# Attention and a gated MLP on one core: the product of the probabilities with V in full fp32, in two 64-column halves of TensorE's array, instead of split fp32r products

## The chip, the cores and the metric

The kernel runs on one core of one Trainium2 chip (trn2). The metric is device time in microseconds (us). TensorE (PE in the profile) multiplies, ScalarE (ACT), VectorE (DVE) and GpSimd (POOL) work on tiles, and SyncE (SP) only issues DMAs.

## What is computed

```python
# q, k, v: [4, 8, 576, 64]; w_in: [512, 2048]; w_out: [2048, 512]
q_rot, k_rot = rotate(q), rotate(k)                 # rotary embedding
scores = q_rot @ k_rot.T / sqrt(64)                 # per head, 576 x 576
attn = exp(scores - rowmax); attn = attn / (rowsum + 1e-9)
x = (attn @ v), heads side by side                  # [2304 tokens, 512]
h = x @ w_in
out = (h * tanh(softplus(h))) @ w_out               # [2304, 512]
```

## The kernel before, in words

**Attention.** The 32 heads go through a software pipeline, one head per step. Each engine works through a list written out by hand (`PE_STEP`, `ACT_STEP`, `DVE_STEP`, `POOL_STEP`). A piece such as `V0-3` is a kind, a number and a shift: in step n it handles head n-3. Each engine takes its pieces strictly in this order, so a piece that waits on a semaphore holds back all that stand behind it.

- On TensorE, K0 to K3 transpose q and k (L566, into `ps_t`). S0 to S4 are the scores of one tile of 128 queries against all keys (L580, four fp32r matmuls of 288 columns, into `ps_s`). T0 to T7 transpose the probabilities (L598, fp32, into one of the three banks of `ps_t`), and V0 to V7 are the product with V (L617, into `ps_pv`).
- On ScalarE, K copies q and k out of `ps_t` (L742), E is the exponential with row sums (L752), and H rounds a transposed group of P to fp32r, `ph` (L764).
- On VectorE, M is the row maximum (L897), L is the remainder `pl` = P - `ph` (L908, and L905 for the last, half-filled key tile), and K copies a part of q and k (L892).
- X copies the product with V from `ps_pv` to `xt`: 256 columns on VectorE (L918), 320 on ScalarE (L774).
- On GpSimd, R is the rotary embedding (L439 to L446), Q splits q and k into two fp32r parts (L452 to L457), C splits V (L466, L468), and B keeps the row sums (L474).

**The product with V.** P and V are each split into two fp32r parts. The two parts of V stand side by side as 128 stationary columns, so one matmul gives the product with both; 18 matmuls (nine of 256 queries, nine of 320) make a head. The part with V's remainder comes out on partitions 64 to 127, both halves go to DRAM, and the MLP adds them up (`sum_x`, L501).

**Banks.** A group T needs a bank of `ps_t` that the third piece before it (of K or T) has been copied out of: `wait_bank`.

**MLP.** Nine blocks of 256 tokens. `load_x` and `load_r` fetch x and the reciprocals of the row sums; GpSimd adds the two halves (L501), scales (L506) and splits (L511, L513); `hidden` is the first product (L681 to L683), `project` the second (L701 to L703). GpSimd's first block comes right behind its last pieces of attention and eight splits of `w_in` (L518, L520).

Of the kernel before, what the change touches and what calls it, by code (L numbers as in the profile page):

```python
# [32 lines left out]
P = 128  # L33
# [5 lines left out]
D = 64  # L39
# [10 lines left out]
LAST_GROUP = (2, 7)  # L50
WIDTH = tuple(len(tiles) * CHUNKS[chunk][1] for chunk, tiles in GROUPS)
GROUP_COL = tuple(sum(WIDTH[:g]) for g in range(NG))
# [4 lines left out]
def order(text):  # L57
# [66 lines left out]
def attention_mlp(nc, q, k, v, w_in, w_out, rope_cos, rope_sin, ident, out):  # L124
# [4 lines left out]
    xt_d = nc.dram_tensor("x_transposed", [2, KC, P, TOKENS], F32).ap()  # L129
# [3 lines left out]
    with ExitStack() as top:  # L133
# [19 lines left out]
        v_hi = sem("v_hi")  # L153
        v_split = sem("v_split")
# [31 lines left out]
        x_summed = sem("x_summed")  # L186
# [46 lines left out]
        v_raw = sb1("v_raw", [P, NT, D])  # L233
        v_st = sb1("v_st", [P, 2, NT, 2, D], F32R)
# [52 lines left out]
        def _(sp):  # L287
# [13 lines left out]
            def load_v(h):  # L301

                if due(h):
                    sp.wait_ge(v_split, h)
                head = v_d[bass.ds(h, 1), :, :]
                sp.dma_start(v_raw[:, 0:4, :],
                             head[:, 0:FULL, :].rearrange("a (t p) d -> p (a t) d", p=P)).then_inc(v_loaded, 16)

                for half in range(2):
                    sp.dma_start(v_raw[half * TAIL:half * TAIL + TAIL, 4, :],  # L310
                                 head[:, FULL:S, :].rearrange("a p d -> p (a d)")).then_inc(v_loaded, 16)

            def store_x(i, e):

                sp.wait_ge(x_taken_v, 2 * i + e + 1)
                sp.wait_ge(x_taken_a, 2 * i + e + 1)
                for a in range(2):
                    dst = xt_d[a, bass.ds(i % 4, 1), e * D:e * D + D, bass.ds((i // 4) * S, S)]
                    sp.dma_start(dst.rearrange("c p s -> (c p) s"), xt[a * D:a * D + D, e, :]
                                 ).then_inc(x_stored[e], 16)  # L320
# [33 lines left out]
            def load_x(b):  # L354

                if due(b):
                    sp.wait_ge(xb_split, b)
                for a, dst in enumerate((x_raw, x_more)):
                    sp.dma_start(dst[:], xt_d[a, :, :, bass.ds(b * TB, TB)].rearrange("c p t -> p c t")
                                 ).then_inc(x_loaded, 16)  # L360

            def load_r(b):

                sp.wait_ge(x_summed, b + 1)
# [37 lines left out]
            sp.wait_ge(pv_done, NG * HEADS)  # L402
# [22 lines left out]
        def _(pool):  # L425
            nc.gpsimd.memset(first[TAIL:P, 0, :, 4, :], 0.0)
            nc.gpsimd.memset(qk_raw[TAIL:P, :, 4, :], 0.0)
            nc.gpsimd.memset(prob[TAIL:P, 0, 4, :], 0.0)
            nc.gpsimd.memset(sums[TAIL:P, :, :], 1.0).then_inc(pads_cleared, 1)
# [30 lines left out]
            def split_v(h, e):  # L460
                pool.wait_ge(v_loaded, 48 * (h + 1))

                if due(NG * (h - 1)):
                    pool.wait_ge(pv_done, NG * (h - 1))
                pool.sem_inc(pool_through, 1)
                nc.gpsimd.tensor_scalar(v_st[:, e, :, 0, :], v_raw[:], 1.0, 1.0, ALU.mult, ALU.mult).then_inc(v_hi, 1)  # L466
                pool.wait_ge(v_hi, h + 1)
                nc.gpsimd.tensor_tensor(v_st[:, e, :, 1, :], v_raw[:], v_st[:, e, :, 0, :].bitcast(F32),  # L468
                                        ALU.subtract).then_inc(v_split, 1)

# [57 lines left out]
            sum_x(0)  # L528
# [3 lines left out]
            with pool.Fori(1, NB) as b:  # L532
                sum_x(b)
# [4 lines left out]
        def _(pe):  # L538
            def wait_bank(slot, n):
# [5 lines left out]
                if kind == "T":  # L545
                    pe.wait_ge(pt_split, NG * head + k + 1)
# [54 lines left out]
            def p_times_v(h, e, g):  # L601
                chunk, tiles = GROUPS[g]
                nq = CHUNKS[chunk][1]
                pe.wait_ge(pt_split, NG * h + g + 1)
                if g == 0:
                    pe.wait_ge(v_split, h + 1)

                if g == 0:
                    if due(h):
                        pe.wait_ge(x_taken_a, h)  # L610
                elif g == 3:
                    pe.wait_ge(x_taken_v, h + 1)
# [17 lines left out]
            def step(i, e):  # L630
                slot = 0
                for kind, k, shift in PE_STEP:
# [13 lines left out]
                    elif real(h):  # L646
                        if kind == "S":
                            scores(h, parity, k)
                        else:
                            p_times_v(h, parity, k)  # L650
# [14 lines left out]
            pe.wait_ge(pt_split, NG * HEADS)  # L665
# [63 lines left out]
        def _(act):  # L729
# [27 lines left out]
            def p_hi(h, g):  # L757
                w, col = WIDTH[g], GROUP_COL[g]
                act.wait_ge(pt_done, NG * h + g + 1)

                if due(h):
                    act.wait_ge(pv_done, NG * (h - 1) + g + 1)
                rows = slice(0, P) if GROUPS[g][1] != (4,) else slice(TAIL, P)
                nc.scalar.activation(ph[rows, col:col + w], ps_t[rows, SLOT_OF["T", g] % NTB, 0:w],  # L764
                                     ACT.Copy).then_inc(pt_hi, 1)

            def take_x(pair, h, e):

                first, nq = CHUNKS[1]
                act.wait_ge(pv_done, NG * h + LAST_GROUP[1] + 1)  # L770

                if due(pair):
                    act.wait_ge(x_stored[e], 32 * pair)
                nc.scalar.activation(xt[:, e, first:first + nq], ps_pv[:, 0:nq], ACT.Copy).then_inc(x_taken_a, 1)  # L774

            def step(i, e):
                for kind, k, shift in ACT_STEP:
                    h, parity = 2 * i + e + shift, (e + shift) % 2
                    if real(h):
# [4 lines left out]
                        elif kind == "H":  # L784
                            p_hi(h, k)
                        else:
                            take_x(i + (e + shift) // 2, h, parity)
# [48 lines left out]
            act.wait_ge(pv_done, NG * HEADS)  # L836
# [25 lines left out]
        def _(dve):  # L862
# [37 lines left out]
            def p_lo(h, g):  # L900
                w, col, bank = WIDTH[g], GROUP_COL[g], SLOT_OF["T", g] % NTB
                dve.wait_ge(pt_hi, NG * h + g + 1)
                if GROUPS[g][1] == (4,):

                    nc.vector.tensor_tensor(ph[0:TAIL, col:col + w], ps_t[TAIL:P, bank, 0:w],  # L905
                                            ph[TAIL:P, col:col + w].bitcast(F32), ALU.subtract).then_inc(pt_split, 1)
                else:
                    nc.vector.tensor_tensor(pl[:, col:col + w], ps_t[:, bank, 0:w],  # L908
                                            ph[:, col:col + w].bitcast(F32), ALU.subtract).then_inc(pt_split, 1)

            def take_x(pair, h, e):

                first, nq = CHUNKS[0]
                dve.wait_ge(pv_done, NG * h + LAST_GROUP[0] + 1)
# [3 lines left out]
                nc.vector.tensor_copy(xt[:, e, first:first + nq], ps_pv[:, 0:nq]).then_inc(x_taken_v, 1)  # L918
# [17 lines left out]
            def step(i, e):  # L936
                for kind, k, shift in DVE_STEP:
                    h, parity = 2 * i + e + shift, (e + shift) % 2
                    if real(h):
# [4 lines left out]
                        elif kind == "L":  # L944
                            p_lo(h, k)
# [3 lines left out]
                    if isinstance(h, int):  # L949
# [4 lines left out]
                        elif kind == "L" and k == 5 and h == HEADS - 1:  # L954
# [86 lines left out]
```

## Time and profile before

| | |
|---|---|
| median of 3 runs | 747.14 us (746.15 to 747.2) |
| the profiled execution | 747.9 us, span of the core 745.9 us |
| TensorE busy | 714.6 us, 96% |
| ScalarE / VectorE / GpSimd busy | 552.6 / 462.1 / 371.3 us |
| mean granted TensorE clock | 0.998 |
| attention | to about 333 us; from 100 to 290 us twenty steps of 9.5 us |
| MLP | from 336.2 us on |

TensorE's matmuls are pipelined, so an entry's duration is longer than the distance to the next one: what a matmul costs in a stream is the distance between starts. The chain of work gives such times directly: each of its pieces ends where the next begins.

### The profile page before, as it was taken

What the parts mean: (1) busy time and instruction counts of PE and PEld (TensorE: products, weight loads), DVE (VectorE), ACT (ScalarE), POOL (GpSimd) and SP (SyncE); (2) the same over time, 40 slices, a digit from 0 to 9 for tenths busy, and PEclk for the clock granted to TensorE, in tenths of its full rate; (3) what the DMA queues carried; (4) which work ended last, traced back from release to release, by engine and by line L of the source; (5) the groups of instructions that cost most, each with busy time, mean ns of one, the idle gap of its engine ahead of it and who ended that gap; (6) DMA issues with size and microseconds to landing.
All of it is one profiled execution on the core that took longest, in us unless ns stands there. A gap on an engine that the chain in (4) does not pass through costs nothing.

```text
span 745.9 us, 16092 instructions
## 1 busy us (share of the span) xinstructions
PE 714.6 (96%) x5098; PEld 666.3 (89%) x5098; DVE 462.1 (62%) x665; ACT 552.6 (74%) x999; POOL 371.3 (50%) x373
## 2 busy tenths in 40 slices
PE   1899999999999999979999999999999999999998
PEld 1799999999999999879899988999988999988996
DVE  4688888888888888975764533343453442533341
ACT  1799999999999999876777576656657557466653
POOL 4999999999999999971411303112030221301000
PEclk9999999999999999999999999999999999999999
DMA  4136633333333333256200201012020200200000
GB/s 86 41 70 194 193 80 78 77 80 79 76 80 81 81 81 81 81 167 222 84 29 29 85 29 58 28 47 66 28 84 0 84 28 28 84 28 0 0 28 28
DMA packets 89956, 52.30 MB, mean 70 GB/s; under 512 B 65456, under 2 KB 79408, under 8 KB 89936
## 3 DMA queue, kind: packets, MB, share of 16 engines
q1 hardware_dynamic: 89936, 52.03, 25.5%
q8 instruction: 12, 0.20, 0.1%
q14 instruction: 8, 0.07, 0.0%
HBM read 37.78 MB, written 14.23 MB: 70 GB/s over the span
## 4 chain that ended last, share of the span: by engine, by line
PE 85%; POOL 6%; issue 3%; DVE 3%; ACT 2%; DMA 1%; SPq 0%; POOLq 0%
PE ps_t L598 10%; PE ps_s L580 9%; PE ps_pv L617 9%; PE ps_h L681 9%; PE ps_y L701 9%; PE ps_h L683 9%; PE ps_h L682 9%; PE ps_y L702 9%; PE ps_y L703 9%; PE ps_t L566 5%; POOL qk_st L457 1%; POOL qk_st L455 1%; POOL win_lo L520 1%; DMA x_more<-reciprocals 1%; DMA sin_t<-rope_sin 0%
## 5 line engine op out<-in xcount | busy, mean ns | idle before, releaser
L989 DVE TENSOR_TENSOR h_sb<-h_sb,m_sb 128x1024 f32<-128x1024 f32 x36 | 57.0, 1583 | 198.5 <-ACT m_sb L823 198.5
L681 PE MATMUL ps_h<-xb_h,win_hi 128*128 128x256 f32 x576 | 163.7, 284 | 2.9 <-POOL xb_l L513 2.9
L682 PE MATMUL ps_h<-xb_l,win_hi 128*128 128x256 f32 x576 | 163.7, 284 | 0.0
L683 PE MATMUL ps_h<-xb_h,win_lo 128*128 128x256 f32 x576 | 163.7, 284 | 0.0
L752 ACT ACTIVATE prob<-ps_s,neg_max 128x576 f32<-128x576 f32 (+1 forms) x160 | 119.0, 743 | 12.9 <-POOL sum_all L474 8.9
L598 PE MATMUL ps_t<-id_f,prob 128*128 128x128 f32 x800 | 125.3, 275 | 0.7 <-DVE rt_early L934 0.3
L897 DVE TENSOR_REDUCE neg_max<-ps_s 128x1 f32<-128x576 f32 (+1 forms) x160 | 119.4, 746 | 5.7 <-PE ps_s L580 5.6
L580 PE MATMUL ps_s<-qkt 128*128 128x288 f32 x640 | 120.6, 311 | 1.9 <-ACT prob L752 1.3
L764 ACT ACTIVATE ph<-ps_t 128x320 fp32r<-128x320 f32 (+3 forms) x256 | 117.6, 473 | 4.8 <-PE ps_t L598 2.5
L681 PEld LDWEIGHTS ps_h<-xb_h,win_hi 128*128 128x128 f32 x576 | 111.2, 193 | 3.8 <-issue 3.2
L701 PE MATMUL ps_y<-wout_hi,gh 128*128 128x512 f32 x288 | 112.4, 390 | 1.0 <-DVE gl L999 1.0
L702 PE MATMUL ps_y<-wout_lo,gh 128*128 128x512 f32 x288 | 112.3, 390 | 0.0
L703 PE MATMUL ps_y<-wout_hi,gl 128*128 128x512 f32 x288 | 112.0, 389 | 0.0
L682 PEld LDWEIGHTS ps_h<-xb_l,win_hi 128*128 128x128 f32 x576 | 111.3, 193 | 0.6
L683 PEld LDWEIGHTS ps_h<-xb_h,win_lo 128*128 128x128 f32 x576 | 111.3, 193 | 0.0
L617 PE MATMUL ps_pv<-ph,v_st 128*128 128x256 f32 (+1 forms) x320 | 106.5, 344 | 2.7 <-DVE xt L918 2.5
L908 DVE TENSOR_TENSOR pl<-ps_t,ph 128x320 fp32r<-128x320 f32 (+1 forms) x192 | 102.9, 551 | 6.2 <-ACT ph L764 0.8
L819 ACT ACTIVATE m_sb<-m_sb 128x1024 f32<-128x1024 f32 x36 | 38.2, 1060 | 90.3 <-DVE m_sb L984 90.3
L511 POOL TENSOR_SCALAR xb_h<-x_raw 128x1024 fp32r<-128x1024 f32 x9 | 9.5, 1054 | 181.2 <-PE ps_h L683 181.0
L598 PEld LDWEIGHTS ps_t<-id_f,prob 128*128 128x128 f32 x800 | 93.7, 140 | 4.8 <-DVE pl L908 0.6
L580 PEld LDWEIGHTS ps_s<-qkt 128*128 128x128 f32 x640 | 92.2, 192 | 3.2 <-ACT prob L752 1.7
L566 PE MATMUL ps_t<-id_r,qk_st 128*128 128x128 f32 x480 | 61.6, 252 | 19.0 <-DVE id_r L884 15.0
(63 smaller groups left out, 1303.8 us busy)
## 6 DMA issues: line engine op xcount, KB each, us to landing
x_transposed<-xt SPq DMA_DIRECT2D x64, 144.0 KB, 2.4
x_raw<-x_transposed SPq DMA_DIRECT2D x9, 512.0 KB, 4.0
x_more<-x_transposed SPq DMA_DIRECT2D x9, 512.0 KB, 4.9
x_more<-reciprocals SPq DMA_DIRECT2D x18, 256.0 KB, 3.8
v_raw<-v_in SPq DMA_DIRECT2D x32, 128.0 KB, 2.2
win_raw<-w_in SPq DMA_DIRECT2D x4, 1024.0 KB, 5.6
wout_raw<-w_out SPq DMA_DIRECT2D x4, 1024.0 KB, 9.4
y_out<-y_sb SPq DMA_DIRECT2D x8, 512.0 KB, 2.8
```

The lines of the kernel that those rows point to most:

```text
L580: mm = nc.tensor.matmul(ps_s[:, buf, part, 0:S // 2], qkt[:, e, stack, t * P:t * P + P], qkt[:, e, 2, part * (S // 2):(part + 1) * (S // 2 ...
L598: mm = nc.tensor.transpose(bank[:, col:col + P], src, id_f[:])
L617: mm = nc.tensor.matmul(ps_pv[:, 0:nq], vT, part[:, col:col + nq], start=(kt == 0 and lo == 0), stop=(kt == 4))
L681: nc.tensor.matmul(o, wh, xb_h[:, c, :], start=(c == 0), stop=False)
L682: nc.tensor.matmul(o, wh, xb_l[:, c, :], start=False, stop=False)
L683: mm = nc.tensor.matmul(o, wl, xb_h[:, c, :], start=False, stop=(c == KC - 1))
L701: nc.tensor.matmul(o, g_h, wout_hi[:, f, :], start=(f == 0), stop=False)
L702: nc.tensor.matmul(o, g_h, wout_lo[:, f, :], start=False, stop=False)
L703: mm = nc.tensor.matmul(o, g_l, wout_hi[:, f, :], start=False, stop=(f == FT - 1))
L752: nc.scalar.activation(prob[0:rows, e, t, :].rearrange("p (a k) -> p a k", a=2), ps_s[0:rows, (5 * e + t) % 2, :, 0:S // 2], ACT.Exp, bias ...
L764: nc.scalar.activation(ph[rows, col:col + w], ps_t[rows, SLOT_OF["T", g] % NTB, 0:w], ACT.Copy).then_inc(pt_hi, 1)
L897: nc.vector.tensor_reduce(neg_max[0:rows, e, t:t + 1], ps_s[0:rows, (5 * e + t) % 2, :, 0:S // 2], AX.XY, ALU.max, negate=True).then_inc(m ...
```

## The change

P stays one fp32 tensor `pt`, and V is loaded from DRAM straight into `v_st`. All V pieces of a head become one, `V0`: for each of five key tiles, two fp32 matmuls with 64 stationary columns, one for queries 0 to 287 (output partitions 0 to 63), one for queries 288 to 575 (partitions 64 to 127). `V0` waits until all eight groups T of its head are copied. Each group is copied once: groups 0 and 5 on ScalarE, the other six on VectorE (all H now). X is one copy of 288 columns on VectorE. C, the second store of x and `sum_x` are gone. The key tile of the last 64 keys has zeros on its first 64 rows of `v_st`.

```diff
-PE_STEP = order("V0-3 K0 V1-3 K1 S1-1 K2 T0-2 K3 V2-3 S2-1 T1-2 V3-3 V4-3 T2-2 S3-1 T3-2 V5-3 T4-2 "
-                "V6-3 S4-1 T5-2 V7-3 T6-2 T7-2 S0")
-ACT_STEP = order("E0 K2+1 H0-1 E1 H1-1 K3+1 H2-1 E2 H3-1 H4-1 E3 H5-1 X1-2 H6-1 E4 H7-1 K0+2")
-DVE_STEP = order("M4-1 L5-2 L6-2 M0 L7-2 K1+1 M1 X0-2 L0-1 M2 L1-1 M3 L2-1 L3-1 L4-1")
-POOL_STEP = order("Q0+3 C0+1 B0 R0+4")
+PE_STEP = order("K0 K1 V0-3 S1-1 K2 T0-2 K3 S2-1 T1-2 T2-2 S3-1 T3-2 T4-2 S4-1 T5-2 T6-2 T7-2 S0")
+ACT_STEP = order("E0 K2+1 H0-1 E1 K3+1 E2 E3 H5-1 E4 K0+2")
+DVE_STEP = order("M4-1 H6-2 M0 H7-2 K1+1 M1 X0-2 M2 H1-1 H2-1 M3 H3-1 H4-1")
+POOL_STEP = order("Q0+3 B0 R0+4")
...
             def step(i, e):
                 n = 2 * i + e
                 if real(n - 2):
                     store_x(i - 1, e)
-                if real(n + 1):
-                    load_v(n + 1)
+                if real(n - 1):
+                    load_v(n - 1, (e - 1) % 2)
...
-            def p_times_v(h, e, g):
...
-                for j, kt in enumerate(tiles):
-                    vT = v_st[:, e, kt, :, :].rearrange("p a d -> p (a d)")
-                    col = GROUP_COL[g] + j * nq
-                    for lo, part in enumerate((ph, pl) if kt < 4 else (ph,)):
-                        mm = nc.tensor.matmul(ps_pv[:, 0:nq], vT, part[:, col:col + nq],
-                                              start=(kt == 0 and lo == 0), stop=(kt == 4))
+            def p_times_v(h, e):
+                wait_taken(h, NG - 1)
+                wait_taken(h, ACT_GROUPS[-1])
+                pe.wait_ge(v_loaded, 32 * (h + 1))
+                if due(h):
+                    pe.wait_ge(x_taken, h)
+                for kt in range(NT):
+                    for side in range(2):
+                        mm = nc.tensor.matmul(ps_pv[side * D:side * D + D, 0:S // 2], v_st[:, e, kt, :],
+                                              pt[:, kt, side * (S // 2):(side + 1) * (S // 2)],
+                                              start=(kt == 0), stop=(kt == 4))
                 mm.then_inc(pv_done, 1)
...
+            def take_p(h, g):
+                chunk, tiles = GROUPS[g]
+                first, nq = CHUNKS[chunk]
+                dve.wait_ge(pt_done, NG * h + g + 1)
+
+                if due(h):
+                    dve.wait_ge(pv_done, h)
+                src = ps_t[:, SLOT_OF["T", g] % NTB, 0:WIDTH[g]].rearrange("p (j q) -> p j q", q=nq)
+                nc.vector.tensor_copy(pt[:, tiles[0]:tiles[-1] + 1, first:first + nq], src).then_inc(pt_taken_v, 1)
```

TensorE, from the end of one step of attention into the next, before (`ps_t<-id_f,prob` are transposes of P, `ps_t<-id_r,qk_st` those of q and k):

```order
L598 MATMUL ps_t<-id_f,prob 128x128 [waits pt_split]
L598 MATMUL ps_t<-id_f,prob 128x128 x2
L580 MATMUL ps_s<-qkt 128x288 [waits exp_done,kt_taken_v,kt_taken_a]
L580 MATMUL ps_s<-qkt 128x288 x3
L617 MATMUL ps_pv<-ph,v_st 128x256 [waits x_taken_a,v_split,pt_split]
L617 MATMUL ps_pv<-pl,v_st 128x256
L617 MATMUL ps_pv<-ph,v_st 128x256
L617 MATMUL ps_pv<-pl,v_st 128x256
L566 MATMUL ps_t<-id_r,qk_st 128x128 [waits qk_parts,pt_split]
L566 MATMUL ps_t<-id_r,qk_st 128x128 x3
```

The same place of the changed kernel:

```order
L574 MATMUL ps_t<-id_f,prob 128x128 [waits pt_taken_v]
L574 MATMUL ps_t<-id_f,prob 128x128 x2
L556 MATMUL ps_s<-qkt 128x288 [waits exp_done,kt_taken_v,kt_taken_a]
L556 MATMUL ps_s<-qkt 128x288 x3
L542 MATMUL ps_t<-id_r,qk_st 128x128 [waits qk_parts,pt_taken_a]
L542 MATMUL ps_t<-id_r,qk_st 128x128 x3
L542 MATMUL ps_t<-id_r,qk_st 128x128 [waits pt_taken_v]
L542 MATMUL ps_t<-id_r,qk_st 128x128 x3
L585 MATMUL ps_pv<-pt,v_st 64x288 [waits v_loaded,x_taken,pt_taken_a,pt_taken_v]
L585 MATMUL ps_pv<-pt,v_st 64x288 x9
L556 MATMUL ps_s<-qkt 128x288 [waits exp_done]
L556 MATMUL ps_s<-qkt 128x288 x3
```

The product with V stood in eight places of the step, each waiting for one group of P; now it stands in one, behind K1, and waits for the last group.

VectorE around the same point, before (the 64-row maximum is M4, the one behind it M0; L905 is the remainder of group 7):

```order
L897 TENSOR_REDUCE neg_max<-ps_s 64x1 [waits s_done]
L908 TENSOR_TENSOR pl<-ps_t,ph 128x320 [waits pt_hi] x2
L897 TENSOR_REDUCE neg_max<-ps_s 128x1 [waits s_done]
L905 TENSOR_TENSOR ph<-ps_t,ph 64x320 [waits pt_hi]
L892 CAST qkt<-ps_t 128x512 [waits s_done,kt_done]
L897 TENSOR_REDUCE neg_max<-ps_s 128x1 [waits s_done]
L918 COPY xt<-ps_pv 128x256 [waits pv_done]
```

and now:

```order
L857 TENSOR_REDUCE neg_max<-ps_s 64x1 [waits s_done]
L868 COPY pt<-ps_t 128x320 [waits pv_done,pt_done]
L857 TENSOR_REDUCE neg_max<-ps_s 128x1 [waits s_done]
L868 COPY pt<-ps_t 128x320 [waits pv_done,pt_done]
L852 CAST qkt<-ps_t 128x512 [waits s_done,kt_done]
L857 TENSOR_REDUCE neg_max<-ps_s 128x1 [waits s_done]
L876 COPY xt<-ps_pv 128x288 [waits pv_done]
```

The last group's piece kept its place behind M0; what waits for it on TensorE has moved.

## Rows read from the trace of the kernel before

**Rows 1.** Busy time of each engine in twenty steps (stretches; columns as headed).

```profile
core 0: us, PE busy (x) PEld busy (x) DVE busy (x) ACT busy (x) POOL busy (x), PEclk, DMA share, GB/s
100.00:290.00 190.00, 188.53 (x1560) 182.05 (x1559) 168.10 (x301) 177.41 (x441) 178.05 (x201) 1.00 0.35 79
```

**Rows 2.** Chain of work: shares of the span, then shares of 100 to 290 us.

```profile
PE 85%; POOL 6%; issue 3%; DVE 3%; ACT 2%; DMA 1%; SPq 0%; POOLq 0%
...
by line: PE ps_t L598 26.3%; PE ps_s L580 25.7%; PE ps_pv L617 24.6%; PE ps_t L566 14.0%; issue 6.9%; POOL qk_st L457 2.5%; POOLq L465 0.1%
```

**Rows 3.** Chain of work in one step: start us, us, what.

```profile
199.64 0.55 PE ps_pv L617 x4
200.19 0.29 PE ps_t L566 x4
...
203.19 0.58 PE ps_pv L617 x4
...
208.10 0.48 POOL qk_st L457
```

**Rows 4.** TensorE in order of time: start us, us, line, what, [idle before, releaser].

```profile
206.63 0.82 PE L598 MATMUL ps_t<-id_f,prob 128*128 128x128 f32 x6
207.21 0.77 PE L580 MATMUL ps_s<-qkt 128*128 128x288 f32 x4
207.82 0.28 PE L617 MATMUL ps_pv<-ph,v_st 128*128 128x256 f32 x1
...
208.17 0.28 PE L617 MATMUL ps_pv<-pl,v_st 128*128 128x256 f32 x1
208.62 0.54 PE L566 MATMUL ps_t<-id_r,qk_st 128*128 128x128 f32 x4 [0.17 <-POOL qk_st L457]
```

**Rows 5.** Groups by shape: count, busy us, mean ns, idle before.

```profile
L617 PEld LDWEIGHTS ps_pv<-ph,v_st 128*128 128x128 f32 x320 | 60.3, 188 | 4.0 <-issue 2.2 <-DVE ph L905 1.3
L908 DVE TENSOR_TENSOR pl<-ps_t,ph 128x320 fp32r<-128x320 f32 x128 | 59.1, 483 | 4.3
L897 DVE TENSOR_REDUCE neg_max<-ps_s 128x1 f32<-128x576 f32 x128 | 95.7, 747 | 4.9 <-PE ps_s L580 4.9
L752 ACT ACTIVATE prob<-ps_s,neg_max 128x576 f32<-128x576 f32 x128 | 95.3, 745 | 12.3 <-POOL sum_all L474 8.9 <-DVE neg_max L897 2.5
L764 ACT ACTIVATE ph<-ps_t 128x512 fp32r<-128x512 f32 x64 | 38.2, 597 | 2.4 <-PE ps_t L598 1.8
```

**Rows 6.** The page's group of all roundings of P on ScalarE.

```profile
L764 ACT ACTIVATE ph<-ps_t 128x320 fp32r<-128x320 f32 (+3 forms) x256 | 117.6, 473 | 4.8 <-PE ps_t L598 2.5
```

**Rows 7.** GpSimd's split of V in order of time.

```profile
208.52 0.47 POOL L466 TENSOR_SCALAR v_st<-v_raw 128x320 fp32r<-128x320 f32 x1
209.07 0.88 POOL L468 TENSOR_TENSOR v_st<-v_raw,v_st 128x320 fp32r<-128x320 f32 x1
```

**Rows 8.** Chain of work from attention into the MLP.

```profile
322.65 2.35 POOL x_raw L501
...
325.76 4.11 DMA x_more<-reciprocals
330.00 2.38 POOL x_raw L506
...
333.69 2.37 POOL xb_l L513
...
337.26 0.21 PE ps_h L682
...
341.05 0.12 PE ps_h L683
```

**Rows 9.** TensorE's first matmul of the MLP in order of time.

```profile
336.20 0.42 PE L681 MATMUL ps_h<-xb_h,win_hi 128*128 128x256 f32 x1 [2.89 <-POOL xb_l L513]
```

**Rows 10.** SyncE's DMA issues in order of time.

```profile
207.72 1.25 SPq L319 DMA_DIRECT2D x_transposed<-xt  x2
210.11 0.40 SPq L306 DMA_DIRECT2D v_raw<-v_in  x1
```

**Rows 11.** DMA issues of 100 to 290 us: count, KB each, median us from issue to landing.

```profile
v_raw<-v_in SPq DMA_DIRECT2D x20, 128.0 KB, 2.2
```

More of the change, by code:

```diff
@@ L49 @@
 NG = len(GROUPS)
-LAST_GROUP = (2, 7)
 WIDTH = tuple(len(tiles) * CHUNKS[chunk][1] for chunk, tiles in GROUPS)
-GROUP_COL = tuple(sum(WIDTH[:g]) for g in range(NG))
+ACT_GROUPS = (0, 5)
 NK = 4
@@ L299, in load_qk, with load_v @@
                                  head[:, FULL:S, :].rearrange("a p d -> p (a d)")).then_inc(loaded, 16)
-            def load_v(h):
-                if due(h):
-                    sp.wait_ge(v_split, h)
+            def load_v(h, e):
+                if due(h - 1):
+                    sp.wait_ge(pv_done, h - 1)
                 head = v_d[bass.ds(h, 1), :, :]
-                sp.dma_start(v_raw[:, 0:4, :],
+                sp.dma_start(v_st[:, e, 0:4, :],
                              head[:, 0:FULL, :].rearrange("a (t p) d -> p (a t) d", p=P)).then_inc(v_loaded, 16)
-                for half in range(2):
-                    sp.dma_start(v_raw[half * TAIL:half * TAIL + TAIL, 4, :],
-                                 head[:, FULL:S, :].rearrange("a p d -> p (a d)")).then_inc(v_loaded, 16)
+                sp.dma_start(v_st[TAIL:P, e, 4, :],
+                             head[:, FULL:S, :].rearrange("a p d -> p (a d)")).then_inc(v_loaded, 16)
             def store_x(i, e):
[L315 to L319, printed above, removed]
+                sp.wait_ge(x_taken, 2 * i + e + 1)
+                for side in range(2):
+                    dst = xt_d[bass.ds(i % 4, 1), e * D:e * D + D, bass.ds((i // 4) * S + side * (S // 2), S // 2)]
+                    sp.dma_start(dst.rearrange("c p s -> (c p) s"), xt[side * D:side * D + D, e, :]
                                  ).then_inc(x_stored[e], 16)
@@ L357, in load_x @@
                     sp.wait_ge(xb_split, b)
-                for a, dst in enumerate((x_raw, x_more)):
-                    sp.dma_start(dst[:], xt_d[a, :, :, bass.ds(b * TB, TB)].rearrange("c p t -> p c t")
-                                 ).then_inc(x_loaded, 16)
+                sp.dma_start(x_raw[:], xt_d[:, :, bass.ds(b * TB, TB)].rearrange("c p t -> p c t")
+                             ).then_inc(x_loaded, 16)
             def load_r(b):
-                sp.wait_ge(x_summed, b + 1)
+                if due(b):
+                    sp.wait_ge(xb_split, b)
                 for e in range(2):
@@ L538, in _, with wait_taken @@
         def _(pe):
+            def wait_taken(head, g):
+                mine = [x for x in range(NG) if (x in ACT_GROUPS) == (g in ACT_GROUPS)]
+                pe.wait_ge(pt_taken_a if g in ACT_GROUPS else pt_taken_v, len(mine) * head + mine.index(g) + 1)
             def wait_bank(slot, n):
@@ L545, in wait_bank @@
                 if kind == "T":
-                    pe.wait_ge(pt_split, NG * head + k + 1)
+                    wait_taken(head, k)
                 elif not real(head):
@@ L599, in p_turn @@
                 mm.then_inc(pt_done, 1)
-            def p_times_v(h, e, g):
[L602 to L612, printed above, removed]
-                for j, kt in enumerate(tiles):
-                    vT = v_st[:, e, kt, :, :].rearrange("p a d -> p (a d)")
-                    col = GROUP_COL[g] + j * nq
-                    for lo, part in enumerate((ph, pl) if kt < 4 else (ph,)):
-                        mm = nc.tensor.matmul(ps_pv[:, 0:nq], vT, part[:, col:col + nq],
-                                              start=(kt == 0 and lo == 0), stop=(kt == 4))
+            def p_times_v(h, e):
[5 more added lines that the diff above has]
+                for kt in range(NT):
+                    for side in range(2):
+                        mm = nc.tensor.matmul(ps_pv[side * D:side * D + D, 0:S // 2], v_st[:, e, kt, :],
+                                              pt[:, kt, side * (S // 2):(side + 1) * (S // 2)],
+                                              start=(kt == 0), stop=(kt == 4))
                 mm.then_inc(pv_done, 1)
@@ L663, in _ @@
                 step(n // 2, n % 2)
-            pe.wait_ge(pt_split, NG * HEADS)
+            wait_taken(HEADS - 1, NG - 1)
+            wait_taken(HEADS - 1, ACT_GROUPS[-1])
             turn_reciprocals(1, range(4), 0)
@@ L755, in exps @@
                                      accum_out=sums[0:rows, e, t:t + 1]).then_inc(exp_done, 1)
-            def p_hi(h, g):
-                w, col = WIDTH[g], GROUP_COL[g]
+            def take_p(h, g):
+                chunk, tiles = GROUPS[g]
+                first, nq = CHUNKS[chunk]
                 act.wait_ge(pt_done, NG * h + g + 1)
                 if due(h):
[L762 to L774, printed above, removed]
+                    act.wait_ge(pv_done, h)
+                src = ps_t[:, SLOT_OF["T", g] % NTB, 0:WIDTH[g]].rearrange("p (j q) -> p j q", q=nq)
+                nc.scalar.activation(pt[:, tiles[0]:tiles[-1] + 1, first:first + nq], src,
+                                     ACT.Copy).then_inc(pt_taken_a, 1)
             def step(i, e):
@@ L898, in row_max, with take_p @@
                                         ALU.max, negate=True).then_inc(max_done, 1)
[L900 to L909, printed above, removed]
+            def take_p(h, g):
+                chunk, tiles = GROUPS[g]
+                first, nq = CHUNKS[chunk]
+                dve.wait_ge(pt_done, NG * h + g + 1)
+                if due(h):
+                    dve.wait_ge(pv_done, h)
+                src = ps_t[:, SLOT_OF["T", g] % NTB, 0:WIDTH[g]].rearrange("p (j q) -> p j q", q=nq)
+                nc.vector.tensor_copy(pt[:, tiles[0]:tiles[-1] + 1, first:first + nq], src).then_inc(pt_taken_v, 1)
             def take_x(pair, h, e):
-                first, nq = CHUNKS[0]
-                dve.wait_ge(pv_done, NG * h + LAST_GROUP[0] + 1)
+                dve.wait_ge(pv_done, h + 1)
                 if due(pair):
                     dve.wait_ge(x_stored[e], 32 * pair)
-                nc.vector.tensor_copy(xt[:, e, first:first + nq], ps_pv[:, 0:nq]).then_inc(x_taken_v, 1)
+                nc.vector.tensor_copy(xt[:, e, :], ps_pv[:, 0:S // 2]).then_inc(x_taken, 1)
             def reciprocals(late):
@@ L953, in step @@
                             take_reciprocals(0)
-                        elif kind == "L" and k == 5 and h == HEADS - 1:
+                        elif kind == "H" and k == 6 and h == HEADS - 1:
                             reciprocals(1)
```

53 lines of the change are left out of this document (15 added, 38 removed).

## The prediction

> **What bounds the kernel now.** I read the busy times of a stretch in the middle of attention first. In twenty steps, 190 us, TensorE is busy for 188.5 us, GpSimd for 178.1, ScalarE for 177.4 and VectorE for 168.1 [rows 1]: four engines within a tenth of each other, with TensorE in front. The chain of work says which of them sets the end. Over the whole span it runs through TensorE for 85% and GpSimd for 6%; in the twenty steps 90.6% of it lies on TensorE and 9.5% on GpSimd's split of q and k and the issue time around it [rows 2]. The order of time shows why: after V's four matmuls TensorE stands still until GpSimd has finished L457, which ends at 208.58, and starts K0 at 208.62 [rows 3, 4]. The last V matmul began at 208.17 and the next instruction could have followed 0.12 us later, so about 0.3 us of a step of 9.5 us is a wait for GpSimd, and the rest is TensorE's own work. The MLP is TensorE's too, and the change leaves its matmuls alone.
>
> So the question is what TensorE's step costs afterwards: its own work, plus waits that stand in its queue.
>
> **TensorE's work.** Of the part of the chain that is on TensorE, the product with V has 24.6 of 90.6 [rows 2]: 0.27 of 9.5 us, or 2.6 us a step. That agrees with pieces of 0.55 and 0.58 us for four matmuls [rows 3]. The other pieces take 9.5 - 2.6 - 0.3 = 6.6 us, and none of them changes.
>
> The trace has no full fp32 product, so the ten new matmuls of 288 columns must be bounded. Four fp32r matmuls of 288 columns, S, take 0.61 us to the next start [rows 4], some 0.13 to 0.15 us each. If a full fp32 matmul cost no more, ten would take 1.3 to 1.5 us. Precision costs passes, though: fp32 transposes of P take 0.58 us for six, 0.097 us each [rows 4], where the fp32r ones of q and k take 0.29 us for four, 0.073 us each [rows 3]. Scaled from 128 to 288 columns, the fp32 price is 0.22 us, and ten make 2.2 us. The upper end is the kernel's own recipe: it gets fp32 from two parts of P times two parts of V, four partial products. Four fp32r products of 0.13 us are 0.53 us for each matmul, ten are 5.3 us; if the two halves run side by side in the array, 2.65 us. Two routes (one after another at the transposes' price, side by side at four products) give 2.2 and 2.65. I take 2.6 us, since the kernel's own way to fp32 needs all four products. The ends are 1.3 and 5.3.
>
> Changing between 128 and 64 columns may empty the array twice a step. A matmul of 0.28 us whose successor starts 0.12 us later [rows 4] overlaps 0.16 us, so this costs at most 0.3 us a step; it goes into the range.
>
> The Trainium skill, "FP8 and Floating Point Precision", TensorE Precision Notes, puts true fp32 at four passes through the array, high and low part of each operand. At 2.4 GHz that would be 4 x 288 columns, 0.48 us; "TensorEngine Tiling (Array Packing)", Theoretical Speedup, gives up to twofold for operands of at most 64 columns, so 2.4 us a head by both rules and 4.8 by the first alone. No row here shows either rule at work on a product.
>
> **What goes away elsewhere.** ScalarE's roundings of P are 117.6 us for 256 [rows 6], of which two of eight groups stay; it also loses X. GpSimd loses 0.47 + 0.88 us a step [rows 7], so it is done with q and k early, and TensorE's 0.3 us wait before K0 goes. All the rest of this relief lies beside TensorE's work and is worth nothing by itself: with ScalarE below 6.5 us and GpSimd near 8 us, TensorE is alone in front.
>
> **The wait that comes in.** V0 waits for H7, the copy of the last group of P, and H7 stands behind M0 on VectorE; M0 needs S0, which TensorE runs after T7. Count from S0's start. S0 takes 0.61 us to issue and ends at 0.77 [rows 4]. M0 takes 0.75, a copy of 320 columns about 0.48 (the nearest row is L908) [rows 5]: H7 is done at 2.0 us. TensorE has S0, K0 and K1 to do, 0.61 + 0.29 + 0.29 = 1.2 us, and stands still for 0.8 us. Before, V7 stood late in the next step and its group had several us. Behind the waiting V0 is everything: S1, and with it M1, E1 and the whole next round, so nothing takes the 0.8 us back.
>
> A smaller one stands before S3, which needs E1. On ScalarE, E1 is behind H0, and H0 needs T0. From S1's start: S1 0.6, K2 0.3, T0 0.4, its end 0.2, H0 0.6 and E1 0.75 [rows 5] are 2.85 us; TensorE has S1, K2, T0, K3, S2, T1 and T2, some 2.6 us. V2, V3 and V4 used to stand between these and cover it; now 0.2 to 0.4 us shows. I take 0.3.
>
> **V's load.** V is now fetched two steps later: on SyncE's queue it stands behind the store of the previous head's x, which needs X, which stands behind M1. From V0's end: S1, M1 and X, 0.77 + 0.75 + 0.48 = 2.0 us; two stores 1.25, two issues of V some 0.4 each [rows 10], gaps together perhaps 0.4; landing 2.2 [rows 11]; about 6.7 us. The next V0 starts 10.3 - 2.6 = 7.7 us after this one's end, so it is hidden, with 1 us to spare. In the last, short steps (head 31) 1 to 2 us of it can show.
>
> **Sum for a step.** 6.6 + 2.6 + 0.8 + 0.3 = 10.3 us against 9.5: +0.8 to 0.9. Steps 3 to 31 have both K and V; the first of them are still filling before and after, so I count 28: +24 us.
>
> **Into the MLP.** Before, GpSimd adds the halves of x (2.35 us), only then are the reciprocals asked for (4.1 us to land), and scaling and splitting run from 330.0 to 336.1 [rows 8]. Without the addition the reciprocals are there early, and the 6 us of splitting can start with the last exponential, which T3 to T7 and V0 of head 31 still follow. TensorE then goes on at once after its last transposes, where it stood still for 2.9 us [rows 9] and then ran at half clock, 0.21 us a matmul instead of 0.12 [rows 8], for about 16 matmuls, 1.5 us. Against these 4.4 us stands head 31's late V. I take -3 us.
>
> Total: 745.9 + 24 - 3 = 767 us of span. The profiled execution's time is 2.0 us above its span and 0.8 above the median, so 768 us for the median. A measurement of this kernel tells 0.2%, 1.5 us, from no change.
>
> **Rivals.**
>
> *The halves run one after another* at four products each: V takes 4.8 to 5.3 us, the step 12.5 to 13.0, +3.0 to +3.5 us for 28 steps, less 3: 828 to 842 us. For it: nothing in the trace shows two matmuls in the array at once, and a weight load of 0.19 us stands before each matmul [rows 5]; if ten of these are not hidden, that alone is 1.9 us. Against it: the two halves share no columns of the array and no partitions of the result, and the trace shows each matmul overlapping its neighbour by more than half of its duration (0.28 us long, 0.12 us apart [rows 4]), so entries behind one another do flow together. The Trainium skill, "TensorE: Matmul & The Clock Gate", The mechanism, says that a weight load overlaps matmuls in flight only where the row groups differ; here both halves use all rows, which speaks for this rival.
>
> *A full fp32 column is cheap* (faster than before): if ten matmuls take 1.3 us, the two waits of 1.1 us still stand, and the step is 6.6 + 1.3 + 1.1 = 9.0, -0.45 us for 28 steps and -3: 731 us. The point from which it decides: V below about 1.6 us a head. For it, the two prices of a transpose, 0.097 against 0.073, are not far apart; with the halves side by side that factor would give 1.1 to 1.3 us.
>
> *The waits are covered.* If VectorE or ScalarE's order lets the waits vanish, V at 2.6 us only replaces V at 2.6, the 0.3 us wait for GpSimd goes, and the time is 735 to 747 us. It needs H7 done within 1.2 us of S0's start, and M0 alone ends at 1.5.
>
> **Chances.** Forecast (V at 2.2 to 3.0 us with its waits) 0.60, giving 755 to 782. One after another 0.22. Cheap fp32 0.13. Waits covered 0.05, mostly faster. Slower 0.82, same 0.03, faster 0.15. The range leaves out the cheap case and reaches over the serial one: 745 to 855.
>
> **What the profile after would show.** TensorE's V matmuls 0.5 us apart in pairs with starts close together (or in a row, for the rival); idle time of about 0.8 us before V0 put down to VectorE's copy L868; GpSimd waiting over 2 us a step; steps of 10.3 us; the MLP beginning without a gap. The prediction is wrong if V's ten matmuls take under 1.6 us or over 3.5, or if V0 does not wait for L868.

## The result: slower by 5.5%, by the forecast mechanism, with almost twice the forecast size

| | before | changed |
|---|---|---|
| median | 747.13 us (746.15 to 747.2) | 787.6 us (786.75 to 788.66) |
| ratio | | 1.0546, 95% interval 1.0527 to 1.0564 |
| span of the profiled run | 745.9 us | 786.9 us |
| a step in the middle of attention | 9.52 us | 10.70 us |
| TensorE's first matmul of the MLP | 336.2 us | 378.3 us |

The forecast was 768 us, +21 us; the measurement is +40.5 us. All of it lies in attention: the MLP begins 42.1 us later and then takes 1 us less.

The busy times of the same stretch as [rows 1], 100 to 290 us of the changed kernel:

```profile
core 0: us, PE busy (x) PEld busy (x) DVE busy (x) ACT busy (x) POOL busy (x), PEclk, DMA share, GB/s
100.00:290.00 190.00, 176.24 (x1421) 147.89 (x1421) 124.76 (x230) 110.92 (x266) 133.21 (x142) 1.00 0.24 55
```

The three other engines lost 43 to 67 us of work in this stretch and are far from full. A part of that is only that fewer steps fit into it, 17.8 in place of 20; counted per step, ScalarE's work fell by 30% and VectorE's and GpSimd's by 16%. TensorE is not full either: 176 us of 190 where it had 188.5. An engine that was the bound now waits. What it waits for stands in the waits of this stretch (who, for whom, us in total, times, longest):

```profile
DVE neg_max L857 <- PE ps_s L556: 63.0, 36, 3.1
ACT qkt L712 <- PE ps_t L542: 60.1, 18, 3.4
POOL qk_st L442 <- PE ps_t L542: 52.4, 18, 3.0
...
PE ps_pv L585 <- DVE pt L868: 13.8, 18, 0.8
```

VectorE, ScalarE and GpSimd each wait some 3 us a step for TensorE, and TensorE waits 0.8 us a step for the copy of P, L868. In order of time, one V0 and what leads to it:

```profile
206.72 0.79 PE L556 MATMUL ps_s<-qkt 128*128 128x288 f32 x4
...
207.35 0.80 PE L542 MATMUL ps_t<-id_r,qk_st 128*128 128x128 f32 x8
207.55 0.76 DVE L857 TENSOR_REDUCE neg_max<-ps_s 128x1 f32<-128x576 f32 x1
...
208.23 0.48 DVE L868 COPY pt<-ps_t 128x320 f32<-128x320 f32 x1
...
208.95 2.65 PE L585 MATMUL ps_pv<-pt,v_st 128*64 128x288 f32 x20 [0.80 <-DVE pt L868]
...
211.53 0.80 PE L556 MATMUL ps_s<-qkt 128*128 128x288 f32 x4
```

S0 starts at 206.72, M0 at 207.55, H7 at 208.23 and ends at 208.71, V0 starts at 208.95. H7 is done 2.0 us after S0's start, as forecast; V0 follows 0.24 us later, which the forecast left out. V0 takes 2.65 us; the next S starts 2.58 us after it. The profile counts 20 entries for ten matmuls: a full fp32 matmul stands there as two instructions with a weight load each. The 20 weight loads of this V0 are busy for 1.61 us and lie inside its 2.65 us, so the rival's price for weight loads that are not hidden (1.9 us) does not show.

Then the end of attention. The last three V0 of the changed kernel, in order of time:

```profile
353.84 4.30 PE L585 MATMUL ps_pv<-pt,v_st 128*64 128x288 f32 x20 [6.69 <-DMA v_st<-v_in]
365.55 2.65 PE L585 MATMUL ps_pv<-pt,v_st 128*64 128x288 f32 x20 [1.86 <-DMA v_st<-v_in]
373.58 4.33 PE L585 MATMUL ps_pv<-pt,v_st 128*64 128x288 f32 x20 [1.80 <-DMA v_st<-v_in]
```

All three wait for V's load, the first for 6.7 us, and two of them take 4.3 us. The forecast had 1 to 2 us for the late load, at head 31 alone; the waits and the slow V0 come to far more. The stretches of the three V0 show why two are slow (the last number but two is the granted clock):

```profile
353.80:358.10 4.30, 4.26 (x21) 2.30 (x21) 0.00 (x0) 0.00 (x0) 0.00 (x0) 0.60 0.44 114
365.50:368.20 2.70, 2.65 (x21) 1.68 (x22) 0.00 (x0) 0.00 (x0) 2.50 (x2) 1.00 0.97 309
...
373.50:377.90 4.40, 4.32 (x21) 2.45 (x22) 0.00 (x0) 2.10 (x5) 0.00 (x0) 0.61 0.00 0
```

The clock granted to the first and the third is 0.60 and 0.61 on average, that is, for most of the stretch the lower level, 1.2 GHz, after waits of 6.7 and 1.8 us. The chain of work up to the first shows how the load came to be late:

```profile
347.31 0.48 DVE pt L868
347.80 0.79 DVE rt_early L892 x2
348.61 0.38 SPq L365
349.03 0.29 SPq L365
349.37 0.29 SPq L365
349.71 0.47 SPq L308
350.22 0.60 SPq L308
350.86 0.59 SPq L298
...
351.51 2.08 DMA v_st<-v_in
...
353.84 0.71 PE ps_pv L585
```

SyncE's program stores the reciprocals of the first 24 heads (L365) at this point, and these are transposed by TensorE just ahead of V0 of head 29. The load of V for that V0 (L298) stands behind the three stores and two stores of x (L308).

### The profile page after: what moved, and what is told of

Its sections match the earlier page's. It is cut to its first block, busy times and chain, and to the rows that moved or that the text cites. A ratio compares the mean times of both kernels' runs of the same rounds, so it can differ in the third digit from the quotient of the medians.

```text
span 786.9 us, 15331 instructions
## 1 busy us (share of the span) xinstructions
PE 731.0 (93%) x5162; PEld 641.2 (81%) x5162; DVE 404.6 (51%) x601; ACT 468.2 (59%) x775; POOL 304.9 (39%) x301
## 4 chain that ended last, share of the span: by engine, by line
PE 84%; DVE 4%; issue 3%; ACT 2%; DMA 2%; POOL 2%; SPq 1%; DVEq 0%; POOLq 0%
PE ps_s L556 12%; PE ps_pv L585 11%; PE ps_t L574 11%; PE ps_y L671 8%; PE ps_y L672 8%; PE ps_y L673 8%; PE ps_h L653 8%; PE ps_h L652 8%; PE ps_h L651 8%; PE ps_t L542 2%; DVE pt L868 2%; DMA v_st<-v_in 1%; DMA sin_t<-rope_sin 0%; DVE gh L955 0%; POOL part_s L431 0%
## 5 line engine op out<-in xcount | busy, mean ns | idle before, releaser
L722 ACT ACTIVATE prob<-ps_s,neg_max 128x576 f32<-128x576 f32 (+1 forms) x160 | 119.0, 744 | 34.1 <-DVE neg_max L857 34.0
L556 PE MATMUL ps_s<-qkt 128*128 128x288 f32 x640 | 126.7, 321 | 1.8 <-ACT prob L722 1.2
L712 ACT ACTIVATE qkt<-ps_t 128x512 fp32r<-128x512 f32 (+1 forms) x96 | 54.3, 566 | 117.9 <-PE ps_t L542 116.2
L585 PE MATMUL ps_pv<-pt,v_st 128*64 128x288 f32 x640 | 88.0, 422 | 32.0 <-DVE pt L868 21.1
L574 PE MATMUL ps_t<-id_f,prob 128*128 128x128 f32 x800 | 115.1, 278 | 0.3 <-ACT pt L735 0.3
L585 PEld LDWEIGHTS ps_pv<-pt,v_st 128*64 128x64 f32 x640 | 52.4, 141 | 55.9 <-issue 30.5
L574 PEld LDWEIGHTS ps_t<-id_f,prob 128*128 128x128 f32 x800 | 90.6, 141 | 8.3 <-DVE pt L868 2.0
L868 DVE COPY pt<-ps_t 128x320 f32<-128x320 f32 (+1 forms) x192 | 90.9, 501 | 0.8 <-PE ps_t L574 0.8
```

What stands on the lines that cost most here:

```text
L556: mm = nc.tensor.matmul(ps_s[:, buf, part, 0:S // 2], qkt[:, e, stack, t * P:t * P + P], qkt[:, e, 2, part * (S // 2):(part + 1) * (S // 2 ...
L574: mm = nc.tensor.transpose(bank[:, col:col + P], src, id_f[:])
L585: mm = nc.tensor.matmul(ps_pv[side * D:side * D + D, 0:S // 2], v_st[:, e, kt, :], pt[:, kt, side * (S // 2):(side + 1) * (S // 2)], start ...
L722: nc.scalar.activation(prob[0:rows, e, t, :].rearrange("p (a k) -> p a k", a=2), ps_s[0:rows, (5 * e + t) % 2, :, 0:S // 2], ACT.Exp, bias ...
L868: nc.vector.tensor_copy(pt[:, tiles[0]:tiles[-1] + 1, first:first + nq], src).then_inc(pt_taken_v, 1)
```

## The experiments

Each ran beside the kernel before; the ratios are to it. Its median was 747.22 us beside four of them (V loaded earlier, H7 first, the halves one after another, all orders changed) and 747.94 us beside the other four, so a difference between one of the first and one of the second four is good to about 1 us.

**V loaded one step earlier.** Head n's V is fetched in SyncE's step n, not n+1, and each of the two buffers has its own semaphore.

```diff
-                if real(n - 1):
-                    load_v(n - 1, (e - 1) % 2)
+                if real(n):
+                    load_v(n, e)
...
-                pe.wait_ge(v_loaded, 32 * (h + 1))
+                pe.wait_ge(v_loaded[e], 32 * (pair + 1))
```

> The changed kernel with each head's V loaded one step earlier on SyncE's queue, with a semaphore for each of the two buffers of V. Theory (the last three heads wait for V): V0 of heads 29, 30 and 31 no longer waits 6.7, 1.9 and 1.8 us for its load, and no V runs at half clock (4.3 us instead of 2.65, twice); about 10 to 12 us less than the changed kernel, 776 us; the steps in the middle stay at 10.7 us. Rival (the loads are late because the DMA queues are full, not because of their place in SyncE's order): under 3 us less.

Measured: 777.44 us (777.2 to 777.74), ratio 1.0403 (1.0386 to 1.042), 10.2 us below the changed kernel. The steps in the middle did not change. The last three V0:

```profile
347.18 2.65 PE L585 MATMUL ps_pv<-pt,v_st 128*64 128x288 f32 x20 [0.70 <-DVE pt L868]
356.29 2.65 PE L585 MATMUL ps_pv<-pt,v_st 128*64 128x288 f32 x20 [0.91 <-DVE pt L868]
364.17 2.65 PE L585 MATMUL ps_pv<-pt,v_st 128*64 128x288 f32 x20 [1.66 <-DVE pt L868]
```

None of them waits for a DMA, and none takes 4.3 us. The load was late by its place in SyncE's order, and the rival of full queues falls. Wait and duration together, head 29 gave back 7.6 us, head 30 1.0 us and head 31 1.8 us.

**H7 ahead of M0** on VectorE:

```diff
-DVE_STEP = order("M4-1 H6-2 M0 H7-2 K1+1 M1 X0-2 M2 H1-1 H2-1 M3 H3-1 H4-1")
+DVE_STEP = order("M4-1 H6-2 H7-2 M0 K1+1 M1 X0-2 M2 H1-1 H2-1 M3 H3-1 H4-1")
```

> The changed kernel with H7 ahead of M0 in VectorE's order, nothing else. Theory (V0 waits for the copy of the last group of P behind M0): the wait of 0.7 to 0.8 us before V0 goes, steps of 10.0 us instead of 10.7, 28 of them, 768 us. Rival (the wait moves: M0 comes 0.5 us later, and with it E0 and the rest of the round): steps stay above 10.4 us, 780 us or more.

Measured: 765.13 us (764.42 to 766.45), ratio 1.0241 (1.0224 to 1.0258), 22.5 us below the changed kernel. In the middle V0 no longer waits; the distance of two V0 is 217.27 - 207.42 = 9.85 us:

```profile
206.01 0.77 PE L556 MATMUL ps_s<-qkt 128*128 128x288 f32 x4
206.62 0.87 PE L542 MATMUL ps_t<-id_r,qk_st 128*128 128x128 f32 x8
207.42 2.65 PE L585 MATMUL ps_pv<-pt,v_st 128*64 128x288 f32 x20
...
217.27 0.95 PE L585 MATMUL ps_pv<-pt,v_st 128*64 128x288 f32 x6
```

One exchange of two pieces on an engine that is idle a third of the time took back more than half of the loss: 0.85 us a step. Two things of the load of V are mixed into the 22.5 us. V0 of head 31 runs at full clock here, 2.65 us in place of 4.33 (only head 29's is still slow, 4.38 us behind a wait of 6.46), and in the first 100 us three V0 now wait for their load, 1.8 us in all, which they do not in the next kernel, with V loaded earlier.

**Both together.**

> load_ahead and h7_first together. If both causes are separate, 777.4 - (787.6 - 765.1) = 755 us and steps of 9.85 us as in h7_first; if the waits of the last heads were partly the same time twice, 757 to 760 us. The distance to reordered (752.5 us) is then what the order on TensorE and ScalarE gives.

Measured: 754.25 us (753.81 to 756.66), ratio 1.0103 (1.0073 to 1.0133), steps of 9.84 us. The gains add up to within 1 us. In part that is chance: head 31's full clock (1.7 us) is gained by either edit alone and so only once by both, and the three early waits of the kernel with H7 first (1.8 us) go only with both.

**The halves one after another.** The loop over the halves outside, the one over key tiles inside; the same ten matmuls.

```diff
-                for kt in range(NT):
-                    for side in range(2):
+                for side in range(2):
+                    for kt in range(NT):
```

> The changed kernel with the two loops of V0 exchanged: five matmuls of the first half of the queries in the first 64 columns, then five of the second half in the others; the same ten matmuls. Theory (a full fp32 matmul of 288 columns takes 0.48 us, and 2.6 us for ten come from two halves side by side): V0 takes 5.0 us instead of 2.6, steps of 13.1 us, 32 times 2.4 us more, 864 us. Rival (nothing runs side by side, ten matmuls cost 0.26 us each one after another): no change, 787 us.

Measured: 834.05 us (833.61 to 835.66), ratio 1.1168 (1.1149 to 1.1187). V0 takes 4.12 us, clearly more than 2.65 and clearly less than the 5.0 of the theory. The first three equal stretches of 0.97 us of one V0 (TensorE's entries of V0 alone; the counts in brackets hold every entry that touches the stretch, and an entry is 0.41 us long):

```profile
207.86:208.83 0.97, 0.97 (x4) 0.57 (x5) 1.00 0.00 0
208.83:209.80 0.97, 0.97 (x7) 0.66 (x7) 1.00 0.59 135
209.80:210.77 0.97, 0.97 (x9) 0.61 (x5) 1.00 0.27 63
```

(The numbers behind the stretch: its length, TensorE busy, its weight loads busy, granted clock, DMA share, GB/s.) Four entries touch the first 0.97 us and start 0.24 us apart; then it is seven and nine. The two answers below count the entries up to 209.3 and up to 209.4 us:

```profile
207.86 1.64 PE L585 MATMUL ps_pv<-pt,v_st 128*64 128x288 f32 x6 [0.80 <-DVE pt L868]
207.86 1.94 PE L585 MATMUL ps_pv<-pt,v_st 128*64 128x288 f32 x8 [0.80 <-DVE pt L868]
```

Two entries start within 0.1 us. In the trace's single records the starts form two rows of ten, each with steps of 0.24 us: one from 207.86 to 210.07, the other from 209.35 on. Ten entries are the five matmuls of one half. So the second half's matmuls began 0.72 us before the last entry of the first half did. The theory's 20 entries in a row were the wrong count for this kernel; the next one makes them follow one another.

**Nine of ten matmuls through the first 64 columns**, in the changed kernel's order.

```diff
+                        half = 1 if side == 1 and kt == 4 else 0
-                        mm = nc.tensor.matmul(ps_pv[side * D:side * D + D, 0:S // 2], v_st[:, e, kt, :],
+                        mm = nc.tensor.matmul(ps_pv[half * D:half * D + D, 0:S // 2], v_st[:, e, kt, :],
...
-                                              start=(kt == 0), stop=(kt == 4))
+                                              start=(kt == 0 and side == 0 or half == 1), stop=(kt == 4))
```

> The changed kernel with nine of V0's ten matmuls writing through the first 64 columns of the array, in the same order; only the last goes through the second half. It leaves out the second half's product: both halves of the queries are summed into one. Theory (each fp32 matmul is two instructions that hold their half of the array for 0.24 us each, and the changed kernel runs two halves side by side): 18 of the 20 instructions now follow one another, 18 x 0.2425 + 0.4 = 4.8 us for V0 instead of 2.65, and it is this overlap that halves_apart kept a part of; 787.6 + 32 x 2.1 = 856 us. Rival (halves_apart lost time through the order of its weights or writes, not through the lack of a neighbour half): V0 stays under 4 us, below 830 us.

Measured: 848.06 us (847.7 to 848.28), ratio 1.1349 (1.1322 to 1.1377). One V0:

```profile
214.94 4.55 PE L586 MATMUL ps_pv<-pt,v_st 128*64 128x288 f32 x20 [0.80 <-DVE pt L869]
```

Its entries are 0.41 us long (the median of 640). If 18 of the 20 follow one another, the start of the last is 17 distances behind the first: (4.55 - 0.41) / 17 = 0.24 us each (the forecast counted 18). For 288 columns at the granted clock of 1.00, 2.4 GHz, 0.24 us is two cycles a column for each entry, and an fp32 matmul has two entries. Two halves side by side take 2.65 us for the same 20 entries. The Trainium skill, "FP8 and Floating Point Precision", TensorE Precision Notes, counts four passes for true fp32; an estimate by that rule is 0.48 us a matmul, and the trace agrees, with 2 x 0.24. The Trainium skill, "TensorEngine Tiling (Array Packing)", Theoretical Speedup, allows up to twofold for 64 columns; here it is 4.55 against 2.65 us, with two entries of the slow form still beside others.

**All orders changed.** V loaded ahead and H7 first as above, V0 moved behind S1, where its group is long copied, K2 ahead of S1, T0 behind S2, and on ScalarE E1 ahead of H0:

```diff
-PE_STEP = order("K0 K1 V0-3 S1-1 K2 T0-2 K3 S2-1 T1-2 T2-2 S3-1 T3-2 T4-2 S4-1 T5-2 T6-2 T7-2 S0")
-ACT_STEP = order("E0 K2+1 H0-1 E1 K3+1 E2 E3 H5-1 E4 K0+2")
+PE_STEP = order("K0 K1 K2 S1-1 V0-3 S2-1 T0-2 K3 T1-2 T2-2 S3-1 T3-2 T4-2 S4-1 T5-2 T6-2 T7-2 S0")
+ACT_STEP = order("E0 K2+1 E1 H0-1 K3+1 E2 E3 H5-1 E4 K0+2")
```

> The changed kernel with V loaded one step earlier, H7 ahead of M0 on VectorE, E1 ahead of H0 on ScalarE, and on TensorE V0 behind S1 (K2 S1 V0 S2 T0 in place of V0 S1 K2 T0 K3 S2). Theory (the slowdown is waits, since V costs what it cost before): TensorE's own work of a step, 6.8 + 2.6 us, is all that is left, steps of 9.5 us as in the kernel before, and with the shorter way into the MLP 742 to 748 us. Rival (the 64-column matmuls cost TensorE more than the split ones, in change-overs too): steps stay above 9.9 us, 760 us or more.

Measured: 752.51 us (750.97 to 753.89), ratio 1.0069 (1.005 to 1.0088). Between the two expectations: the best form of the change, and still slower than before. Its stretch and its chain of work over it:

```profile
100.00:290.00 190.00, 189.66 (x1560) 156.35 (x1557) 140.38 (x253) 123.75 (x292) 146.55 (x155) 1.00 0.27 62
```

```profile
by line: PE ps_t L574 31.0%; PE ps_s L556 30.0%; PE ps_pv L585 26.4%; PE ps_t L542 12.4%; issue 0.2%
```

TensorE is busy for 189.7 of 190 us by the profile, and the chain never leaves it. But the ends of matmuls are modelled, and they cover a wait that the weight loads show (who, for whom, us in total, times, longest, from 100 to 290 us):

```profile
PEld ps_t L574 <- ACT pt L735: 5.1, 20, 0.3
```

Once a step a weight load between T1 and T2 stands still for 0.25 us until ScalarE has copied group 0 of P, which now stands behind E1. So the wait before V0 is gone, and a short one has come in. A step is 9.7 us (V0 at 205.73 and 215.43), or 9.75 us on the average of the steps in the middle:

```profile
205.73 2.65 PE L585 MATMUL ps_pv<-pt,v_st 128*64 128x288 f32 x20
208.30 0.79 PE L556 MATMUL ps_s<-qkt 128*128 128x288 f32 x4
...
215.43 2.65 PE L585 MATMUL ps_pv<-pt,v_st 128*64 128x288 f32 x20
```

**V0 in two lumps**, on the kernel above: key tiles 0 and 1 before S2, 2 to 4 behind it.

```diff
-PE_STEP = order("K0 K1 K2 S1-1 V0-3 S2-1 T0-2 K3 T1-2 T2-2 S3-1 T3-2 T4-2 S4-1 T5-2 T6-2 T7-2 S0")
+PE_STEP = order("K0 K1 K2 S1-1 V0-3 S2-1 V1-3 T0-2 K3 T1-2 T2-2 S3-1 T3-2 T4-2 S4-1 T5-2 T6-2 T7-2 S0")
...
-                for kt in range(NT):
+                for kt in ((0, 1), (2, 3, 4))[k]:
...
```

> The kernel reordered with V0 cut in two: key tiles 0 and 1 before S2, tiles 2 to 4 behind it; the same matmuls. Theory (changing between 128 and 64 columns costs TensorE time: 0.70 us from the start of S to V0 where S to its next neighbour is 0.61, and 0.34 us from V's last start to S where its own are 0.24 apart): one more pair of changes a step, about 0.2 to 0.4 us, 32 steps, 759 to 765 us. Rival (a change-over is free and the extra time of reordered's steps is elsewhere): no change, 752.5 us.

Measured: 760.51 us (759.69 to 761.19), ratio 1.0176 (1.015 to 1.0202); 8.0 us, or 0.25 us for each of 32 heads, above the kernel with one lump. The steps in the middle are 0.3 us longer, and the one short wait before T2 is the same in both kernels (4.8 us in 19 times here). So one more visit to the 64-column form costs a quarter of a microsecond or a little more beside its matmuls, and the form with one lump should pay as much once a step.

With it the steps can be added up. Before, a step of 9.5 us was 9.2 us of TensorE's work and a wait of 0.3. In the kernel with all orders changed, 9.75 us less 0.25 for the visit and 0.25 for the wait leave 9.2 or 9.3 us: the work with V in full fp32 costs what it cost split, to within 0.1 us a step, the visit is new, and the wait for ScalarE stands in place of that for GpSimd. Taking this wait away too would be worth up to 28 x 0.25 = 7 us, an estimate that no run here tests.

**H7 on ScalarE**, on the reordered kernel.

```diff
-ACT_GROUPS = (0, 5)
+ACT_GROUPS = (0, 5, 7)
...
-ACT_STEP = order("E0 K2+1 E1 H0-1 K3+1 E2 E3 H5-1 E4 K0+2")
-DVE_STEP = order("M4-1 H6-2 H7-2 M0 K1+1 M1 X0-2 M2 H1-1 H2-1 M3 H3-1 H4-1")
+ACT_STEP = order("E0 K2+1 E1 H0-1 K3+1 E2 E3 H5-1 E4 H7-1 K0+2")
+DVE_STEP = order("M4-1 H6-2 M0 K1+1 M1 X0-2 M2 H1-1 H2-1 M3 H3-1 H4-1")
...
-                wait_taken(h, ACT_GROUPS[-1])
+                wait_taken(h, NG - 2)
```

> The kernel reordered with the copy of the last group of P on ScalarE behind E4 instead of on VectorE ahead of M0. In the middle TensorE has no waits left, so steps stay at 9.7 us; the waits of 0.9 and 2.1 us before V0 of heads 30 and 31, where VectorE copies six groups in a row, should fall by about 0.5 us each. About 751.5 us; a rival has ScalarE as busy there as VectorE: no change.

Measured: 758.96 us (757.41 to 759.27), ratio 1.0151 (1.0123 to 1.0178): 6.5 us worse. At the end it did what was expected, waits of 1.3 and 0.5 us in place of 0.9 and 2.1. But the steps in the middle are 10.0 us: behind E4, H7 ends late, and now one of K0 to K2 waits 0.2 us a step (3.9 us in 19 times), since its bank is freed by it. The chain of work of the stretch leaves TensorE again:

```profile
by line: PE ps_pv L585 25.8%; PE ps_s L556 21.7%; PE ps_t L574 20.1%; PE ps_t L542 11.3%; issue 9.8%; DVE neg_max L857 3.6%; DVE pt L868 3.5%; ACT pt L735 1.6%; ACT prob L722 1.1%; DVEq L927 0.6%; DVEq L866 0.4%; ACTq L702 0.2%; DVEq L856 0
```

The expectation looked at ScalarE's busy time and not at the place in its queue.

## Why the prediction was right, and where its sizes were off

**The bound** was TensorE, with a small wait for GpSimd: right. The change took 30% of a step's work off ScalarE and 16% off VectorE and GpSimd. GpSimd's 0.3 us wait before K0 went, as forecast; beyond that nothing came of it.

**V's price** was taken as 2.6 us, unchanged from [rows 2, 3], by "two halves side by side, four products each": 2.65 us, shown by the two experiments that take the neighbour half away (4.12 and 4.55 us). The number is better founded by them than by the prediction, which chose between two routes that happened to lie close together (2.2 and 2.65). They also set the rival of halves one after another where it would have been, 848 us or above, with the terms below that the forecast had too small; its forecast range was 828 to 842. What the prediction held for that rival, that weight loads overlap matmuls in flight only where the row groups differ, does not hold in this trace: both halves use all rows, and a V0's weight loads, busy for 1.61 us, lie beside its matmuls. The rival of a cheap fp32 column falls: a column costs two cycles in each of two instructions. The prediction's point from which the change would gain, V below 1.6 us, is 1.9 us by its own terms: 9.5 - 6.6 - 1.1 = 1.8, and the 3 us on the way into the MLP add 0.1. With 2.65 measured nothing hangs on it.

**The wait before V0** was forecast as 0.8 us; the profile shows 0.8, and without it each step is 0.85 us shorter and the kernel 22.5 us faster. This term was right. The smaller wait before S3, for E1, was taken as 0.3 us and is 0.2: in the stretch from 100 to 290 us the weight loads of S wait 3.8 us for L722, in 18 times.

**The change-over** was priced at "at most 0.3 us a step" and then left out of the sum. It should have been in it: 0.25 us. A second small term is missing too. T5 to T7 and their nine matmuls take 1.10 us from start to start in the changed kernel (205.62 to 206.72) and 0.92 in the one with all orders changed, and between them a weight load waits 0.15 us for VectorE's copy of P; no experiment took this wait away by itself. Own work 9.2, V0's wait 0.8, S3's 0.2, the change-over 0.25 and this 0.2 are 10.65 of the 10.7 us measured. Over 28 steps the forecast had 24 us and 33 were measured.

**V's load** was forecast hidden "with 1 us to spare", 1 to 2 us showing at head 31. In the middle it is hidden. At the end it cost 10.2 us. Head 31 took 1.8 us of it. That is the forecast's size, met by luck: it is slow matmuls and no added wait, since with V loaded early the V0 of head 31 waits as long, 1.7 us, for VectorE. What was missed is head 29, 7.6 us, and 1.0 us at head 30. The count of the way through SyncE's queue took the steady step; at head 29 three stores of reciprocals stand in the queue, which wait for a transpose just ahead of the V0 that needs the load. Behind the wait of 6.7 us V0 then ran mostly at the lower clock level, 1.65 us more. This is the term that was mis-sized most against its own size.

**Into the MLP**, -3 us: in the kernel with V loaded ahead the MLP's first matmul comes at full rate right behind the last transposes, and no wait for GpSimd is left, as forecast. Of the 42.1 us by which the changed kernel's MLP starts later, 33 are 28 steps of 1.18 us and 10 the late loads; what remains, -1 us, holds this gain and the late start of the first V0, which were not measured apart.

## What to carry to other kernels

Relief on engines that are not the bound was worth nothing here beyond the one short wait that it ended; when a product is moved from many small places into one lump, ask which copy it now waits for last and what stands ahead of that copy in its engine's queue. A full fp32 product in 64-column halves cost the same here as the split fp32r one with 128 columns, because the halves run side by side, and a visit to the other form of the array cost a quarter of a microsecond. A TensorE that the profile shows as busy throughout can still wait: look at the waits of its weight loads. Count a DMA's way through the issuing queue at the ends of a pipeline too: an unrelated store there that waits for the consumer's own engine makes the load late by the whole way.

## What the runs showed that was not expected

- A full fp32 matmul stands in the profile as two entries with a weight load each. Entries on one 64-column half are 0.24 us apart at 288 columns, and those of the two halves run side by side: 20 in 2.65 us.
- With the five matmuls of one half written ahead of the five of the other, V0 took 4.12 us and not 5.0: near the seam matmuls of the second half started while earlier ones of the first half were still to come. In the kernel with nine of ten matmuls on one half, the last matmul of the program is the one on the other half; the record of it that raises the semaphore `pv_done` starts at 218.65, and two more of the same V0 start after it, at 218.84 and 219.08. The ends of matmuls are modelled, so whether they also end out of order was not seen.
- V0 of head 31 ran at a mean granted clock of 0.61 behind a wait of 1.80 us, that of head 30 at 1.00 behind one of 1.86 us. The length of the wait alone does not tell the two apart.
